# Retention's loads in two chains, small and spread zero matmuls, tiles inside turns, differences of x first at the end

## Time and profile before

| what | value |
|---|---|
| median of 3 runs | 622.18 us |
| profiled execution | 622.52 us, its span 620.7 us |
| PE busy | 605.9 us (98% of the span) |
| ACT, DVE, POOL busy | 234.7, 264.0, 278.2 us |
| mean granted PE clock | 0.989 |
| instructions | 9829 |

### The profile page before, as it was taken

How to read it: one execution, slowest core, us unless ns; L and a number is a source line. 1 busy time by engine, 2 the same in 40 slices (tenths; PEclk the granted TensorE clock), 3 DMA queues, 4 the chain that set the end, 5 groups by cost and what they waited for, 6 DMA issues and landing times.

```text
span 620.7 us, 9829 instructions
## 1 busy us (share of the span) xinstructions
PE 605.9 (98%) x4016; PEld 547.0 (88%) x4016; DVE 264.0 (43%) x361; ACT 234.7 (38%) x434; POOL 278.2 (45%) x230
## 2 busy tenths in 40 slices
PE   6799999999999999999999999999999999999997
PEld 4699799999999999999999999989989999989996
DVE  2467654423154434154534154535545432324334
ACT  2464433322323332223432123435455454334431
POOL 2658645535335544435552535532446553443300
PEclk9699999999999999999999999999999999999999
DMA  8963202332112331112322112321211232201002
GB/s 345 331 213 109 80 35 68 104 101 68 35 35 68 103 103 57 46 35 68 102 84 62 58 34 69 102 69 37 67 34 49 69 105 84 68 1 52 1 1 101
DMA packets 24923, 50.47 MB, mean 81 GB/s; under 512 B 2864, under 2 KB 2992, under 8 KB 24880
## 3 DMA queue, kind: packets, MB, share of 16 engines
q1 hardware_dynamic: 24736, 49.84, 25.1%
q10 hardware_dynamic: 144, 0.02, 0.0%
HBM read 47.49 MB, written 2.36 MB: 80 GB/s over the span
## 4 chain that ended last, share of the span: by engine, by line
PE 92%; DVE 2%; ACT 2%; issue 1%; DMA 1%; POOL 1%; SPq 0%
PE bank L494 30%; PE bank L496 29%; PE bank L495 29%; PE bank L442 1%; DMA loaded<-in_feats 1%; PE bank L470 1%; PE bank L612 1%; PE bank L474 1%; ACT xt L736 0%; ACT w_hi L368 0%; DVE acc_sb L888 0%; DVE acc_sb L892 0%; POOL w_lo L395 0%; DVE xs_a L962 0%; DVE xs_a L959 0%
## 5 line engine op out<-in xcount | busy, mean ns | idle before, releaser
L395 POOL TENSOR_TENSOR w_lo<-w_raw,w_hi 128x512 fp32r<-128x512 f32 x96 | 134.6, 1416 | 149.8 <-ACT w_hi L368 149.8
L494 PE MATMUL bank<-w_hi,h_hi 128*128 128x512 f32 x432 | 168.7, 391 | 0.0
L496 PE MATMUL bank<-w_hi,h_lo 128*128 128x512 f32 x432 | 168.3, 390 | 0.0
L495 PE MATMUL bank<-w_lo,h_hi 128*128 128x512 f32 x432 | 168.3, 390 | 0.0
L875 DVE TENSOR_TENSOR h_act<-part,bank 128x384 f32<-128x384 f32 x96 | 52.9, 551 | 169.9 <-PE bank L496 169.4
L390 POOL TENSOR_TENSOR ws<-ws_f,ws 128x1024 fp32r<-128x1024 f32 x24 | 57.6, 2401 | 145.1 <-ACT ws L364 145.1
L496 PEld LDWEIGHTS bank<-w_hi,h_lo 128*128 128x128 f32 x432 | 81.1, 188 | 16.9
L495 PEld LDWEIGHTS bank<-w_lo,h_hi 128*128 128x128 f32 x432 | 81.1, 188 | 12.3
L494 PEld LDWEIGHTS bank<-w_hi,h_hi 128*128 128x128 f32 x432 | 81.0, 188 | 12.1
L722 ACT ACTIVATE part<-bank 128x384 f32<-128x384 f32 x72 | 35.3, 491 | 138.6 <-PE bank L496 138.6
L842 DVE SCALAR_TENSOR_TENSOR h_lo<-h_act,h_hi 128x384 fp32r<-128x384 f32 x64 | 73.2, 1153 | 20.5 <-ACT h_hi L712 19.9
(11 more groups left out here) (88 smaller groups left out, 863.0 us busy)
## 6 DMA issues: line engine op xcount, KB each, us to landing
w_raw<-in_weights SPq DMA_DIRECT2D x144, 256.0 KB, 2.7
loaded<-in_toks SPq DMA_DIRECT2D x9, 512.0 KB, 7.0
loaded<-in_feats SPq DMA_DIRECT2D x8, 512.0 KB, 6.2
out<-acc_sb SPq DMA_DIRECT2D x6, 256.0 KB, 2.1
out<-acc_sb SPq DMA_DIRECT2D x1, 768.0 KB, 3.5
loaded<-in_first SPq DMA_DIRECT2D x1, 726.0 KB, 4.4
ident<-in_ident SPq DMA_DIRECT2D x1, 64.0 KB, 5.0
p_nat<-in_probs ACTq DMA_DIRECT2D x1, 18.0 KB, 5.1
```

Of the source, the lines that this page charges most:

```text
L395: pool.tensor_tensor(w_lo[layer][:, x], w_raw[:, r % RAW], w_hi[layer][:, x].bitcast(F32), ALU.subtract).then_inc(s_wl, 1)
L494: pe.matmul(out, w[0], x[0], start=first, stop=False, **more)
L495: pe.matmul(out, w[0], x[1], start=False, stop=False, **more)
L496: return pe.matmul(out, w[1], x[0], start=False, stop=last, **more)
```

## The change

- SP: `feats(c)` is now issued only when `feats(c-1)` has landed, `toks(c)` only when `toks(c-1)` has landed, from chunk 2 on; one weight load stands behind each.
- PE: the 7 zero matmuls of 128x512 at the start become 72 of 64x64 (`small_zeros`), the 5 after the first scores become 4; 4, 4 and 3 zeros of 128x512 stand ahead of turns 1, 2 and 3, and 2 more inside turns 1 and 2.
- PE: tiles 0, 3, 4 and 6 move into the middle of turns 3, 5, 6 and 7 (`TILE_AMID`, between `scores_and_state` and `output`); tiles 1, 2, 5 and 7 stay after turns 3, 4, 6 and 8 (`TILE_AFTER`).
- Weight jobs stand in other turns; the row tables of DVE (`rows`) are made earlier; after the turns DVE makes `full[0]` and `full[1]` before tile 7's low part, and the last `first_lo` in the middle; POOL waits for all four `t_lo` before its next weight jobs; ACT does the two jobs of stage 1 between `t_hi(0, 1)` and `t_hi(0, 2)`.

```diff
-TILES_IN = {3: (0,), 4: (1,), 5: (2, 3), 6: (4,), 7: (5, 6), 8: (7,)}
+TILE_AMID = {3: 0, 5: 3, 6: 4, 7: 6}
+TILE_AFTER = {3: 1, 4: 2, 6: 5, 8: 7}
-ROWS_IN = {4: 5, 5: 6, 6: 7, 7: 8}
+ROWS_IN = {0: (2, 3), 1: (4, 5), 2: (6,), 3: (7, 8)}
-WARM_START, WARM_NEXT = 7, 5
+SMALL, FIRST, AHEAD, AMID = 72, 4, {1: 4, 2: 4, 3: 3}, {1: 2, 2: 2}
...
             load_toks(0)
-            for c in range(1, SLOTS):
-                load_feats(c)
-                load_toks(c)
+            load_feats(1)
+            load_toks(1)
+            feats_there(1)
+            load_feats(2)
+            toks_there(1)
+            load_toks(2)
+            feats_there(2)
+            load_feats(3)
+            load_weights(0)
+            toks_there(2)
+            load_toks(3)
+            at = 1
             for c in range(SLOTS, PLACES):
+                feats_there(c - 1)
                 sp.wait_ge(s_o, c - SLOTS + 1)
                 load_feats(c)
+                load_weights(at)
+                toks_there(c - 1)
                 load_toks(c)
+                load_weights(at + 1)
+                at += 2
...
+            def small_zeros(count):
+                for _ in range(count):
+                    pe.matmul(banks[7][HALF[0], 0:CH], zeros[:, 0:CH], zeros[:, 0:CH], start=True, stop=True)
...
-            keep_warm(WARM_START)
+            small_zeros(SMALL)
...
-            keep_warm(WARM_NEXT)
+            keep_warm(FIRST)
             for c in range(PLACES):
+                keep_warm(AHEAD.get(c, 0))
                 if has_state(c):
                     scores_and_state(c)
+                keep_warm(AMID.get(c, 0))
+                if c in TILE_AMID:
+                    early_tile(TILE_AMID[c])
                 output(c)
-                for t in TILES_IN.get(c, ()):
-                    s, i = divmod(t, ITEMS)
-                    plain_ready(s, i)
-                    plain_products(s, i, range(KT))
+                if c in TILE_AFTER:
+                    early_tile(TILE_AFTER[c])
...
             for n in range(4):
                 t_hi(0, n)
-            for job in IN_STAGE[1]:
-                job_hi(act, job)
+                if n == 1:
+                    for job in IN_STAGE[1]:
+                        job_hi(act, job)
...
+            dve.wait_ge(s_xt, PLACES)
             dve.tensor_tensor(full[0], b12, b11, ALU.subtract).then_inc(s_tf, 1)
-            dve.tensor_tensor(full[2], b22, b12, ALU.subtract).then_inc(s_tf, 1)
             dve.wait_ge(s_tf, 1)
             dve.tensor_tensor(full[1], b22, full[0], ALU.subtract).then_inc(s_tf, 1)
-            dve.wait_ge(s_tf, 3)
+            plain_lo(*divmod(TILE_AFTER[PLACES - 1], ITEMS))
+            dve.tensor_tensor(full[2], b22, b12, ALU.subtract).then_inc(s_tf, 1)
+            t_lo(0, 0)
+            first_lo(PLACES - 1)
+            dve.wait_ge(s_tf, 2)
             dve.tensor_tensor(full[3], full[1], b21, ALU.subtract).then_inc(s_tf, 1)
...
+            pool.wait_ge(s_tl, 4)
             for s in range(1, ALL_STAGES):
```

More of the change, by code:

```diff
@@ L53 @@
 STATE_BANK, OUT_BANK = 2, 3
-TILES_IN = {3: (0,), 4: (1,), 5: (2, 3), 6: (4,), 7: (5, 6), 8: (7,)}
[L57 to L61, removed]
-ROWS_IN = {4: 5, 5: 6, 6: 7, 7: 8}
+TILE_AMID = {3: 0, 5: 3, 6: 4, 7: 6}
+TILE_AFTER = {3: 1, 4: 2, 6: 5, 8: 7}
+JOBS_IN = {2: (("w1", 0, 0),), 3: (("w1", 0, 1), ("w1", 0, 2)), 4: (("w1", 0, 3), ("w1", 0, 4)),
+           5: (("w1", 0, 5), ("w1", 0, 6)), 6: (("w1", 0, 7), ("w2", 0, 0), ("w2", 0, 1)),
+           7: (("w2", 0, 2), ("w2", 0, 3), ("s", 0, 0)), 8: (("w2", 0, 4), ("w2", 0, 5))}
+ROWS_IN = {0: (2, 3), 1: (4, 5), 2: (6,), 3: (7, 8)}
 PROBS_IN = 5
-WARM_START, WARM_NEXT = 7, 5
+SMALL, FIRST, AHEAD, AMID = 72, 4, {1: 4, 2: 4, 3: 3}, {1: 2, 2: 2}
 STAGES = 6
@@ L415, in _, with feats_there, toks_there @@
             sp.dma_start(loaded[:, lead - CONSTS:lead + 2 * KIND], first_in).then_inc(s_feats[0], 16)
+            def feats_there(c):
+                sp.wait_ge(s_feats[c % SLOTS], landed(c))
+            def toks_there(c):
+                sp.wait_ge(s_toks[c % SLOTS], landed(c))
             load_toks(0)
-            for c in range(1, SLOTS):
-                load_feats(c)
-                load_toks(c)
-            at = 0
+            load_feats(1)
[10 more added lines that the diff above has]
+            at = 1
             for c in range(SLOTS, PLACES):
-                for r in range(at, at + WEIGHTS_IN[c - SLOTS]):
-                    load_weights(r)
-                at += WEIGHTS_IN[c - SLOTS]
+                feats_there(c - 1)
                 sp.wait_ge(s_o, c - SLOTS + 1)
                 load_feats(c)
+                load_weights(at)
+                toks_there(c - 1)
                 load_toks(c)
+                load_weights(at + 1)
+                at += 2
             sp.dma_start(ident[:, :], ident_in).then_inc(s_id, 16)
@@ L522, in plain_products, with early_tile @@
                     mm.then_inc(s_l1, 1)
+            def early_tile(t):
+                s, i = divmod(t, ITEMS)
+                plain_ready(s, i)
+                plain_products(s, i, range(KT))
             def product(s, j):
@@ L734, in t_hi @@
                 i = T_ORDER[n]
-                act.wait_ge(s_tf, (9, 8, 6, 10)[n] if e else (3, 2, 1, 4)[n])
+                act.wait_ge(s_tf, (9, 8, 6, 10)[n] if e else (2, 3, 1, 4)[n])
                 act.activation(x_sum(i, 0), x_full(e, i), ACT.Copy).then_inc(s_th, 1)
@@ L740, in _ @@
                     first_hi(c - 1)
-                for t in TILES_IN.get(c - 1, ()):
-                    plain_hi(*divmod(t, ITEMS))
+                if c - 1 in TILE_AFTER:
+                    plain_hi(*divmod(TILE_AFTER[c - 1], ITEMS))
                 if has_state(c):
@@ L753, in _ @@
                         job_hi(act, job)
+                if c in TILE_AMID:
+                    plain_hi(*divmod(TILE_AMID[c], ITEMS))
             for n in range(4):
                 t_hi(0, n)
-            for job in IN_STAGE[1]:
-                job_hi(act, job)
+                if n == 1:
+                    for job in IN_STAGE[1]:
+                        job_hi(act, job)
             for s in range(2, ALL_STAGES):
@@ L937, in _ @@
                     masked(c)
-                if c == 0:
-                    for i in range(2, 5):
-                        rows(i)
                 if c > 0:
@@ L946, in _ @@
                     first_lo(c - 1)
[L947 to L950, removed]
+                for i in ROWS_IN.get(c, ()):
+                    rows(i)
+                if c - 1 in TILE_AFTER and c < PLACES:
+                    plain_lo(*divmod(TILE_AFTER[c - 1], ITEMS))
                 if c == PROBS_IN + 1:
                     probs()
-            first_lo(PLACES - 1)
+                if c in TILE_AMID:
+                    plain_lo(*divmod(TILE_AMID[c], ITEMS))
             b11, b21 = xf[:, 0:KH, 0:TC], xf[:, KH:, 0:TC]
@@ L958, in _ @@
             full = [x_full(0, i) for i in range(4)]
+            dve.wait_ge(s_xt, PLACES)
             dve.tensor_tensor(full[0], b12, b11, ALU.subtract).then_inc(s_tf, 1)
-            dve.tensor_tensor(full[2], b22, b12, ALU.subtract).then_inc(s_tf, 1)
             dve.wait_ge(s_tf, 1)
             dve.tensor_tensor(full[1], b22, full[0], ALU.subtract).then_inc(s_tf, 1)
-            dve.wait_ge(s_tf, 3)
+            plain_lo(*divmod(TILE_AFTER[PLACES - 1], ITEMS))
[3 more added lines that the diff above has]
+            dve.wait_ge(s_tf, 2)
             dve.tensor_tensor(full[3], full[1], b21, ALU.subtract).then_inc(s_tf, 1)
-            dve.wait_ge(s_tf, 4)
-            for n in range(4):
+            for n in range(1, 4):
                 t_lo(0, n)
```

## The result

The changed kernel takes 626.03 us (median of 4 runs, 625.21 to 627.51) against 622.38 us before: ratio 1.0065, 95% interval 1.0049 to 1.0081. It is slower by 3.7 us. The forecast was 617.3 us, the range 614.5 to 620.8. Its profiled execution took 626.43 us with a span of 624.7.

A forecast was written before the change was run, and what follows sets the result against it. The prediction took PE as the bound, idling early on late instruction blocks. From 622.52 us, 5.6 gained by turn 4, 1.8 lost at turn 8 and 1.1 gained at the end gave 617.6, median 617.3; range 614.5 to 620.8.

The forecast's parts named there:

- waits for blocks of 256 instructions: PE's stalls of 2.29, 2.74 and 1.64 us in `of_state` were read as late instruction blocks.
- Tile 0 became bound by POOL: Behind turn 3's scores, tile 0 awaits its weights' low part on POOL: start at 21.8 us, end at 24.1.
- tile 1 by `toks` 5: Tile 1 waits for `v_decay(5)` and its job until 25.7 us, ends at 28.0, when turn 4 starts.
- rival B: Clock falls once in turns 2 or 3, tile 0 takes 4.06 us: 619.2 to 621.0 us; chance 0.16.
- Turn 8: New PE stall ahead of `output(8)`, which needs `decayed(7)`: 1.8 us, between 0.9 and 2.5.
- The end: After the turns, the new order of DVE and ACT work removes PE's gap ahead of P6: gain 1.12 us.
- the pace of the chains: Early loads: the queue stays full behind the first links, 3.9 us a chunk, `toks` 5 at 23.3 us.
- the sum: Profiled execution: 622.52 - 5.6 + 1.8 - 1.1 = 617.6 us, 0.3 above the median.
- Rival C: Slower: chains leave the DMA engines empty; 5.5 us a chunk eats everything, 6.5 gives 625.5 us; chance 0.06.
- Zeros. I charge nothing.: The zeros in the opening and around turns 1 to 3 stand where PE waits anyway: no cost.
- block 193 is asked for earlier: With 72 small zeros, record 193 falls into the first scores at 6.1 us, not at 8.5.
- the tiles in the turns counted as a gain: Turn 4 starts at 28.0 us, not 31.06, with one tile (2.3 us) more behind it: part of 5.6 us gain.

The follow-up runs named there:

- experiment 2: Kernel before with only the two chains of loads added: 624.56 us, ratio 1.0042.
- experiment 1: Changed kernel with the loads issued as in the kernel before, all else as changed: 621.96 us, ratio 1.0006 to the kernel before.
- experiment 4: Kernel before with only the new zeros, in the opening and around turns 1 to 3: 626.30 us, ratio 1.0061.
- experiment 5: Kernel before with only the opening changed, 72 small zeros in place of 7 large ones: 626.57 us, ratio 1.0062.
- experiment 12: Kernel before plus: tiles, end, zeros in turns, 623.37 us; tiles, end, opening of 72 then 4, 622.55; end, zeros in turns, 622.03.
- experiment 10: Kernel before with the changed tiles and end, but tile 6 behind `output(7)` again: 623.51 us, ratio 1.0030.
- experiment 3: Kernel before with loads waiting one landing further back than the two chains, about 1.5 MB in flight: 623.04 us, ratio 1.0012.
- experiment 6: Kernel before with the opening as 36 zero matmuls of 64x128, 58 instructions more than before: 623.89 us, ratio 1.0030.

## Why the prediction was wrong, step by step

**Right.** The stalls of PE are waits for blocks of 256 instructions; five kernels with other counts ahead of the turns moved them by as much. With the two chains a block came sooner in turns 1 to 3 (experiment 2). The three stalls in `of_state` went. Tile 0 became bound by POOL behind the landing of `toks` 4, tile 1 by `toks` 5. The clock stayed at full through turns 1 to 3, down to half only when PE stood still ahead of tile 0. That made tile 0 3.98 us long, as in rival B, but cost nothing: PE then waited another 0.55 us for tile 1's low part. Turn 8: forecast 1.8 us, measured 1.37, since ACT began `h_hi` about 0.2 us sooner than I had it and PE ended `output(7)` about 0.2 later. The end: forecast 1.1, measured 1.8 (1.28 up to P6 and 0.56 behind it, which I had not looked for).

**The step that failed first: the pace of the chains.** "3.9 us a chunk", with `toks` 5 at 23.3 us and turn 4 at 28.0. Measured: `toks` 2 to 5 released POOL at 13.58, 19.07, 25.35 and 31.02, 5.8 us a chunk; turn 4 at 35.64, 7.6 us late, of the 8.8 us by which the profile missed the sum. `toks` 8 released POOL at 46.34, where I had chunk 8 down at 35. I took 1.85 us as the whole cost of a link, from a lone 256 KB, and compared it with 2.6 us of transfer in flight. In the trace, `feats` 2 was issued at 7.88 and landed at 11.86: 3.98 us, where 1.85 + 1.3 makes 3.15. That is an early link; from 13.6 to 31 us the landings of `toks` came 5.5 to 6.3 us apart. The rate of 259 GB/s against 382 says the same. Rival C had the mechanism (though the DMA engines were not empty but 0.84 busy), a break-even of 5.5 us a chunk and a chance of 0.06; measured 5.8. It should have had far more: its row of 226 GB/s stood among my own, and I used it for the case against the forecast only. The chains account for about 4 us (experiment 1) in the changed kernel.

**The second: "Zeros. I charge nothing."** I had counted the 130 instructions for one purpose, that block 193 is asked for earlier, and not for the other, that all later block starts come 130 instructions earlier in the work as well. By my own pace of 4.5 to 6.3 us for 256 they were worth 2.3 to 3.2 us. Alone they cost 4.1 to 4.6 us (experiments 4 and 5), in the profile of experiment 5 at one block start between two tiles, with the half clock behind it. In the changed kernel, where landings bind as well, 1.8 us. (The zeros in the turns are 4 + 4 + 3 and 2 + 2, thus 15, where the prediction and the expectations count 17; nothing hangs on it.)

**The third: the tiles in the turns counted as a gain.** I gave tile 1's earlier place its full 2.3 us and priced one new wait. With loads and zeros of before they cost 3.6 us, 1.4 of it at turn 8, which I had, and 2.0 at block starts in turns 5 and 6: I had not followed the blocks beyond turn 4.

Every kernel of this study has waits at block starts while loads are on the way, the longest of each 0.8 to 4.0 us. Later, with about 25 us of matmuls to a block, neither kernel shows one. The Trainium skill (Runtime: NRT & Kernel Launch, Instruction fetch mechanics) says that crossing a block is "mostly hidden"; the traces disagree with it in the first 52 us and agree later.

The parts do not add up, for each hides behind the other: chains, zeros and end alone give +2.4, +4.1 and -1.9 us, and the tiles with the end +1.8; the whole change gave +3.7. The profiles fit that in each the landing or the block bound, whichever came last.

## What to carry to other kernels

Count instructions, not only their time: where an engine runs through many tiny ones while loads fill the DMA queues, its own instructions arrive late, every 256 of them, and each instruction added ahead (a warm-up of zeros too) moves all later block starts. What that costs depends on whether a long piece of work, as a tile here, still lies between one block start and the next; 130 instructions cost 4.6 us in one order of the tiles and none in another (experiments 5 and 12). A load that waits for a landing on the issuing engine pays more than the fixed latency of a lone transfer; keep more in flight than one link's issue-to-landing time, and measure the rate before building on it. When a change repairs one wait, follow the path to its end and price what is late next with its margin, for the wait may only move (experiment 10).

## What the runs showed of the hardware

- PE's instructions come in blocks of 256. One block's packet is 0.02 MB and takes about 1.07 us; PE went on 1.4 to 1.5 us after its end (in the kernel before and in experiment 5).
- From a block start to the next block's use it took 5.6 to 6.7 us in the stretches with 393 to 411 GB/s of loads (kernel before, experiments 1, 3, 5, 6 and others). At lower rates the rate does not tell it: 4.3 us at 337 GB/s (experiment 2), 4.8 at 329 (before), but 6.0 at 350 and 5.8 at 160 (experiment 5).
- The rate of the loads by what is in flight, 8 to 24 us: 382 GB/s (four chunks), 349 (1.5 MB), 285 (1.0 MB or less) in the kernel before, 259 in the changed kernel with the same chains.
- Full clock over turns 1 to 3 brought nothing by itself: at a granted clock of 1.00 from 19.1 to 30.1 us the kernel with the zeros in the turns and the new end took 622.03 us, against 620.23 without these zeros.
